# Reordering the start of the second mixture in a three-stage kernel: turns, logits, row tables and gates

## The reference, cut to what matters

```python
x = attention(...)                       # 2304 tokens x 512
x = routed_mixture(x)                    # each token: the one expert of 8 with the greatest logit
# second mixture: every token goes through all 8 experts (512 -> 1024 -> 512)
logits = x @ w_gate
P = np.exp(logits - logits.max())
for _ in range(8):                       # eight rounds of row and column scaling ("Sinkhorn")
    P /= P.sum(1, keepdims=True) + 1e-09
    P /= P.sum(0, keepdims=True) + 1e-09
    P *= N / E
for e in range(E):
    out += P[:, e:e + 1] * (np.maximum(x @ w1[e], 0.0) @ w2[e])
```

## Time and profile before

| | |
|---|---|
| time, median of 3 runs | 2225.56 us (2223.52 to 2228.18) |
| profiled execution, its time | 2224.41 us |
| profiled execution, its span | 2222.8 us |
| busy: PE, DVE, ACT, POOL | 2122.7, 1475.5, 903.0, 760.2 us |
| mean granted TensorE clock | 0.979 |
| last routed output to the end of step 2 | 643.57 to 804.6 us |

### The profile page before, as it was taken

How to read it: one execution, slowest core, us unless ns; L and a number is a source line. 1 busy time by engine, 2 the same in 40 slices (tenths; PEclk the granted TensorE clock), 3 DMA queues, 4 the chain that set the end, 5 groups by cost and what they waited for, 6 DMA issues and landing times.

```text
span 2222.8 us, 36560 instructions
## 1 busy us (share of the span) xinstructions
PE 2122.7 (95%) x12117; PEld 1937.3 (87%) x12117; DVE 1475.5 (66%) x2842; ACT 903.0 (41%) x2042; POOL 760.2 (34%) x646
## 2 busy tenths in 40 slices
PE   7998996999997899999999999999999999999998
PEld 6888886899987799998998899988998899988997
DVE  7877774876655766666666666666666666666663
ACT  5666652555544233333333333333333333333331
POOL 3544530111244323332334233322334333323331
PEclk9999997999998999999999999999999999999999
DMA  4322202777633212221123212222122222212220
GB/s 99 103 73 61 67 2 94 246 230 224 223 106 100 76 43 72 76 76 58 58 76 99 63 58 76 76 67 67 57 76 91 66 63 77 76 61 65 66 77 29
DMA packets 158031, 192.98 MB, mean 87 GB/s; under 512 B 76976, under 2 KB 76976, under 8 KB 157872
## 3 DMA queue, kind: packets, MB, share of 16 engines
q1 hardware_dynamic: 151472, 169.99, 25.5%
q0 software_dynamic: 6400, 20.98, 2.7%
HBM read 172.04 MB, written 18.87 MB: 86 GB/s over the span
## 4 chain that ended last, share of the span: by engine, by line
PE 78%; DVE 3%; issue 1%; DMA 1%; ACT 0%; another core or an unknown queue 0%; SPq 0%; POOL 0%; DVEq 0%; ACTq 0%; POOLq 0%
PE b_pso L1489 12%; PE b_pso L1490 12%; PE b_pso L1491 12%; PE b_psp L1435 10%; PE b_psp L1438 10%; PE b_psp L1437 10%; PE b_pso L961 2%; PE b_pso L963 2%; PE b_pso L962 2%; PE b_psp L963 2%; PE b_psp L961 2%; PE b_psp L962 2%; PE b_psl L1413 1%; PE b_pst L1359 0%; PE b_pst L1370 0%
## 5 line engine op out<-in xcount | busy, mean ns | idle before, releaser
L1283 POOL TENSOR_TENSOR b_w2l<-b_w2r,b_w2h 128x512 fp32r<-128x512 f32 x192 | 242.4, 1297 | 911.7 <-ACT b_w2h L1582 911.5
L1435 PE MATMUL b_psp<-b_x,b_ah 128*128 128x384 f32 x1344 | 454.7, 338 | 6.4 <-DVE b_u3c L1896 6.4
L1489 PE MATMUL b_pso<-b_w2h,b_hh 128*128 128x512 f32 x1152 | 450.7, 391 | 10.0 <-DVE b_acc L1935 9.0
L1438 PE MATMUL b_psp<-b_x,b_al 128*128 128x384 f32 x1344 | 452.5, 337 | 0.0
L1437 PE MATMUL b_psp<-b_x,b_ah 128*128 128x384 f32 x1344 | 452.1, 336 | 0.0
L1491 PE MATMUL b_pso<-b_w2h,b_hl 128*128 128x512 f32 x1152 | 450.8, 391 | 0.0
L1490 PE MATMUL b_pso<-b_w2l,b_hh 128*128 128x512 f32 x1152 | 450.7, 391 | 0.0
L1935 DVE SCALAR_TENSOR_TENSOR b_acc<-b_pso,b_prob,b_acc 128x512 f32<-128x512 f32 x264 | 198.0, 750 | 287.0 <-PE b_pso L1491 282.7
L1616 ACT ACTIVATE b_p<-b_psp 128x384 f32<-128x384 f32 x96 | 46.5, 484 | 577.5 <-PE b_psp L1438 577.4
L1489 PEld LDWEIGHTS b_pso<-b_w2h,b_hh 128*128 128x128 f32 x1152 | 217.5, 189 | 55.7 <-DVE b_acc L1935 9.9
L1435 PEld LDWEIGHTS b_psp<-b_x,b_ah 128*128 128x128 f32 x1344 | 254.5, 189 | 10.9 <-DVE b_u3c L1896 7.0
(11 more groups left out here) (276 smaller groups left out, 3892.8 us busy)
## 6 DMA issues: line engine op xcount, KB each, us to landing
dense_raw<-in_moe_w SPq DMA_DIRECT2D x192, 256.0 KB, 4.1
b_w2r<-in_moe_w SPq DMA_DIRECT2D x192, 256.0 KB, 2.7
weights_raw<-in_moe_w SPq DMA_DIRECT2D x176, 256.0 KB, 3.6
y_sorted<-r_y POOLq DMA_DIRECT2D x22, 256.0 KB
weights_raw<-in_q SPq DMA_DIRECT2D x32, 128.0 KB, 2.4
weights_raw<-in_k SPq DMA_DIRECT2D x32, 128.0 KB, 2.5
weights_raw<-in_v SPq DMA_DIRECT2D x32, 128.0 KB, 2.4
x_tokens<-a_xs SPq DMA_DIRECT2D x4, 1024.0 KB, 4.2
```

The costliest lines, as they stand in the source:

```text
L1283: g_.tensor_tensor(w2l[:, j, :], w2r[:, j, :], w2h[:, j, :].bitcast(F32), ALU.subtract).then_inc(s_wl, 1)
L1435: t_.matmul(bank, ah[:, i, d, col], bh[i][:, d, :], start=(first and d == 0), stop=False, skip_group_check=True)
L1438: m = t_.matmul(bank, al[:, i, d, col], bh[i][:, d, :], start=False, stop=(d == CH - 1), skip_group_check=True)
L1489: t_.matmul(o, hh[:, f, tok], w2h[:, f, :], start=(q == 0), stop=False)
```

## The change

Step by step: (1) `rows_chain` is cut into eight pieces inside `r_first(1)`, `mark_rows` into marks in groups 2 and 3, the table's 20 matmuls stand inside group 3's output, and `row_tables` runs a group later; for this groups 2 to 4 are written out instead of looped. (2) Tiles 0 to 5 are scaled by DVE (`first_scaled`), before its `r_ahead(last)`, and no longer by POOL. (3) The first six logits stand between the matmuls of the last routed output. (4) All seven splits of step 0 stand ahead of the last two copies to `y`; block T3 of the first pass gets memory of its own (`p1u2`), so that it needn't wait for the logits. (5) Turns and logits of tiles 6 to 17 begin at unit 14, step 0's first output tile, and end at unit 26; greatest is at 28, exp at 31, rows at 33, and the Sinkhorn rounds at 34, 36, 38, 54, 56, 58, 74, 76, all after output tiles. (6) The gates are first needed at k = 4: steps 2 and 3 add up in `acc2` (the memory of `xt[0]`), which k = 5 merges. (7) POOL does `sums(1)` ahead of the last eight fetches. (8) ACT's splits for the next step are spread over the output tiles as DVE's are.

```diff
+        acc2 = xt[0][:].rearrange("p c w -> p (c w)").rearrange("p (t d) -> p t d", d=DM)
...
         for j in range(NT - TP):
-            extras.setdefault(j + 1, []).append(("turn", TP + j))
-            extras.setdefault(j + 2, []).append(("logits", TP + j))
-        extras.setdefault(15, []).append(("greatest", 0))
-        for it in range(8):
-            extras.setdefault(19 + 4 * it, []).append(("sinkhorn", it))
+            extras.setdefault(14 + j, []).append(("turn", TP + j))
+            extras.setdefault(15 + j, []).append(("logits", TP + j))
+        extras.setdefault(28, []).append(("greatest", 0))
+        extras.setdefault(31, []).append(("exp", 0))
+        extras.setdefault(33, []).append(("rows", 0))
+        for it, u in enumerate((34, 36, 38, 54, 56, 58, 74, 76)):
+            extras.setdefault(u, []).append(("sinkhorn", it))
...
+        SPLIT_AT = (0, 1, 2), (3,), (4,), (5,), (6,), ()
...
             for t in range(TP):
                 fetch(t)
-            for t in range(TP):
-                scaled(t)
             store(last2)
             sums(0)
             store(last)
...
             w2_lo(0)
+            sums(1)
             for t in range(TP + RING, NT):
                 fetch(t)
-            sums(1)
...
-            pe.wait_ge(s_tm, 7)
-            table(psi, hotr, rows_of, NT * NV).then_inc(s_tf, 1)
-            with pe.Fori(2, last) as g:
+            def rows_table(m, f):
+                if m == 0 and f == 2 * FC - 2:
+                    pe.wait_ge(s_tm, 7)
+                    table(psi, hotr, rows_of, NT * NV).then_inc(s_tf, 1)
+
+            def first_logits(m, f):
+                if f in (1, 3, 5):
+                    logits(m * GT + f // 2)
+
+            for g in range(2, 5):
+                r_output(g - 1, g - 2, True, rows_table if g == 4 else None)
+                r_hidden(g)
+            with pe.Fori(5, last) as g:
                 r_output(g - 1, g - 2, True)
                 r_hidden(g)
             r_output(last2, count(pe, 3), True)
             r_hidden(last, last2)
-            for t in range(TP):
-                logits(t)
-            r_output(last, last2, False)
+            r_output(last, last2, False, first_logits)
...
                 for j in range(2):
                     hidden(k, j)
-                if k + 1 < STEPS:
-                    for i in range(7):
-                        if (k + 1) % (2 * E) == 0:
-                            x_hi((k + 1) // (2 * E), i)
-                        w1_hi(k + 1, i)
                 for t in range(TP):
+                    if k + 1 < STEPS:
+                        for i in SPLIT_AT[t]:
+                            if (k + 1) % (2 * E) == 0:
+                                x_hi((k + 1) // (2 * E), i)
+                            w1_hi(k + 1, i)
                     fill(k, 14 + t)
...
-                    dve.wait_ge(s_lg, TP * (p + 1))
+                    if p:
+                        dve.wait_ge(s_lg, TP * (p + 1))
...
+            def first_scaled(t):
+                dve.wait_ge(s_yg[t], 16)
+                v_.tensor_scalar(acc[:, t, :], acc[:, t, :], row_gate[:, t:t + 1], None, ALU.mult).then_inc(s_x0, 1)
...
-                if k == 2:
+                into = acc2 if k in (2, 3) else acc
+                if k == 4:
                     dve.wait_ge(s_k, 3 + 7 * 8)
                     dve.wait_ge(s_acc, TP + t + 1)
                     v_.tensor_scalar(acc[:, t, :], acc[:, t, :], prob[:, at, 0:1], None, ALU.mult).then_inc(s_sc, 1)
                     dve.wait_ge(s_sc, t + 1)
+                elif k == 5:
+                    dve.wait_ge(s_acc, TP * 4 + t + 1)
+                    v_.scalar_tensor_tensor(out=acc[:, t, :], in0=acc2[:, t, :], scalar=prob[:, at, 1:2],
+                                            in1=acc[:, t, :], op0=ALU.mult, op1=ALU.add).then_inc(s_sc, 1)
+                    dve.wait_ge(s_sc, TP + t + 1)
...
             r_first(0)
-            rows_chain()
             r_ahead(1, 0, True)
-            r_first(1, mark_rows)
+            r_first(1, rows_chain)
+            r_ahead(2, 1, True)
+            r_first(2, mark_in_tile)
+            r_ahead(3, 2, True)
+            r_first(3, mark_tile)
+            r_ahead(4, 3, True)
             row_tables()
-            with dve.Fori(2, last) as g:
+            r_first(4)
+            with dve.Fori(5, last) as g:
                 r_ahead(g, g - 1, True)
                 r_first(g)
+            for t in range(TP):
+                first_scaled(t)
             r_ahead(last, count(dve, 2), True)
             r_first(last)
             for i in range(7):
...
                 x_lo(0, i)
                 w1_lo(0, i)
-                if i == 2:
-                    r_ahead(count(dve), last, False)
+            r_ahead(count(dve), last, False)
             scaled(TP)
```

More of the change, by code:

```diff
@@ L1387, in r_hidden, with r_output @@
                         turn(f)
-            def r_output(g, before, turn_next):
+            def r_output(g, before, turn_next, also=None):
                 for m in range(RT):
@@ L1405, in r_output @@
                             f == 0, f == 2 * FC - 1)
+                        if also is not None and f < 2 * FC - 1:
+                            also(m, f)
                     i.then_inc(s_ro, 1)
@@ L1615, in hidden @@
                 after(act, s_add, 5 * (n - 1) + 1)
-                a_.activation(p1[:], bank_a, ACT.Copy).then_inc(s_p1, 1)
+                if n == 0:
+                    act.wait_ge(s_bl, T3 + 1)
+                a_.activation(p1, bank_a, ACT.Copy).then_inc(s_p1, 1)
                 if j == 0:
@@ L1718, in sources @@
                 v_.tensor_copy(idx[:, FT:], idxf[:]).then_inc(s_idx, 1)
[L1720 to L1749, removed]
-                v_.tensor_scalar(row_i[:, 1], row_i[:, 0], 7, None, ALU.logical_shift_right)
-                v_.tensor_scalar(row_i[:, 2], row_i[:, 0], P - 1, None, ALU.bitwise_and).then_inc(s_tc, 1)
-                dve.wait_ge(s_tc, 9)
-                v_.tensor_copy(row_f[:], row_i[:, 1:3]).then_inc(s_tc, 1)
@@ L1827, in extra @@
                     v_.tensor_reduce(pmax, prob[:].rearrange("p t e -> p (t e)"), AX_X, ALU.max).then_inc(s_k, 1)
+                elif kind == "exp":
                     dve.wait_ge(s_am, 1)
                     v_.tensor_scalar(nmax, amax, -1.0, None, ALU.mult).then_inc(s_k, 1)
+                elif kind == "rows":
                     dve.wait_ge(s_e, 1)
@@ L1881, in hidden @@
                 after(dve, s_add, 5 * n)
-                v_.tensor_tensor(u2[:], bank_b, p1[:], ALU.add).then_inc(s_add, 1)
+                v_.tensor_tensor(u2, bank_b, p1, ALU.add).then_inc(s_add, 1)
                 fill(k, 7 * j + 1)
@@ L1889, in hidden @@
                     dve.wait_ge(s_bl, 7 * (k // (2 * E) + 1))
-                v_.tensor_tensor(u3, bank_c, u2[:], ALU.add).then_inc(s_add, 1)
+                v_.tensor_tensor(u3, bank_c, u2, ALU.add).then_inc(s_add, 1)
                 fill(k, 7 * j + 3)
@@ L1901, in hidden @@
                 after(dve, s_hl, 4 * (n - 1) + 3)
-                v_.tensor_tensor(c21, bank_c, u2[:], ALU.add).then_inc(s_add, 1)
+                v_.tensor_tensor(c21, bank_c, u2, ALU.add).then_inc(s_add, 1)
                 hidden_lo(n, 2, c22, 2 + j, b)
@@ L1907, in hidden @@
                 after(dve, s_hl, 4 * (n - 1) + 4)
-                v_.tensor_tensor(c12, bank_d, u2[:], ALU.add).then_inc(s_add, 1)
+                v_.tensor_tensor(c12, bank_d, u2, ALU.add).then_inc(s_add, 1)
                 hidden_lo(n, 3, c21, 2 + j, a)
@@ L1925, in added @@
                 o = pso[:, t % 2, :]
-                if k == 0:
-                    v_.tensor_copy(acc[:, t, :], o).then_inc(s_acc, 1)
-                elif k == 1:
-                    v_.tensor_tensor(acc[:, t, :], o, acc[:, t, :], ALU.add).then_inc(s_acc, 1)
+                if k in (0, 2):
+                    v_.tensor_copy(into[:, t, :], o).then_inc(s_acc, 1)
+                elif k in (1, 3):
+                    v_.tensor_tensor(into[:, t, :], o, into[:, t, :], ALU.add).then_inc(s_acc, 1)
                 elif e == 0 and half == 0:
@@ L1965, in _ @@
                     if k + 1 < STEPS:
-                        for i in ((0, 1, 2), (3,), (4,), (5,), (6,), ())[t]:
+                        for i in SPLIT_AT[t]:
                             if (k + 1) % (2 * E) == 0:
```

69 lines of the change are left out of this document (54 added, 15 removed).

## The result

The changed kernel takes 2213.2 us (median of 4 runs, 2210.43 to 2214.93) against 2226.87 us (4 runs, 2223.52 to 2228.53) for the kernel before. The ratio is 0.9939, with a 95% interval of 0.9922 to 0.9957: 13.7 us faster, where 18.4 were forecast. Timed again later, on another occasion, it took 2214.81 us (10 runs) against 2218.79 (19 runs), a ratio of 0.998 (0.997 to 0.999), that is 4.0 us faster. The two intervals don't overlap: the size of the gain over the kernel before isn't settled between 4 and 14 us. The changed kernel had moved by 1.6 us, the kernel before by 8.1.

A forecast was written before the change was run, and what follows sets the result against it. PE, busy in 95% of the span, was taken as the bound, so gains must come from its idle time or lower clock. 18.2 - 0.3 + 4.0 - 3.5 = 18.4 us faster, 2207 us; range 2200.5 to 2215.5.

The forecast's parts named there:

- Part 1: Table work in groups 1 to 3: PE's idle stretches of 1.37 and 2.67 us hide behind PE, gain 4.0 us.
- Part 2: First scaling on DVE ahead of the last group: PE's gap grows to about 3.6 us, clock 1.5, together 3.5 lost.
- Part 3: First logits inside the last routed output: it takes 16.2 us at the upper clock and ends 4.9 us earlier.
- Part 4: Hidden part of step 0: PE's stall before A22 is 7.8 us instead of 11.3, released by DVE's addition into u3.
- rival B: Step 0's ring scaling held by POOL's fetches and w2_lo: A22 starts at 678.8, gain 12.4 us, 2213; chance 0.15.
- rival D: Whole kernel, no difference: all upper bounds of cost at once leave 4.6 us of gain; chance 0.06.
- Part 5: Turns and logits in output 0 and hidden 1: twelve pairs of 1.28 us, each of the two stages 23.2 us.
- Part 6: Output 1: a new wait behind POOL's all-reduce (0.5 us) and w2_lo(1), PE stalling before the third tile; 5.5 us lost.
- Part 7: Sinkhorn rounds in output parts: steps 1 and 2 lose their gaps of 3.2 us; step 2 takes 31.4 us.
- A: Output 1 hardly stalls, 1.5 us instead of 5.5, as DVE runs ahead of POOL's sums: gain 22.4, 2203; chance 0.13.
- C: Small matmuls between large ones hold TensorE at its lower clock to the end of hidden 1: slower, 2274; chance 0.03.
- E: Output 1: DVE and POOL exclude each other for whole instructions, 8.5 us lost, gain 15.4, 2210; chance 0.13.

The follow-up runs named there:

- two of the single repairs: Changed kernel with w2_lo(1) and sums(2) ahead of POOL's all-reduce, 2206.22 us; changed kernel with only the six first scalings moved into DVE's idle slot, 2209.2 us.

## Why the prediction was right or wrong

The net at the end of step 2 is 804.6 - 790.22 = 14.4 us; the forecast had 18.7 there (18.2 + 4.0 - 3.5), and 18.4 behind step 3. Three stretches add up to it:

| stretch | forecast | measured |
|---|---|---|
| to the marker | +4.0 | 614.20 - 606.37 = +7.8 |
| marker to last routed output | -3.5 | 29.4 - 32.6 = -3.2 |
| last routed output to end of step 2 | +18.2 | 161.0 - 151.3 = +9.8 |

The time lay inside the stated range, but partly by luck: the stage that the change rearranges won 8.4 us less than forecast, 5.6 of them in output 1, and the stretch to the marker won 3.8 more, of which 2.3 have nothing to do with the change (part 1).

**Part 1** was right in its mechanism and a little low. The gaps are gone, and the table's 20 matmuls, at home between other matmuls, cost 1.2 us of the group's period instead of the 2.6 that they took alone. From the first turn of group 1 to the marker it is 211.5 us (394.91 to 606.37) instead of 217.0 (397.17 to 614.20), 5.6 less: the two gaps, 4.0, and the rest from the matmuls and the clock beside them. The experiment that undid it gives 6.2 us in the trace and 5.8 in the timing. The prediction had left the table's matmuls at no gain. The other 2.3 of the 7.8 are 1.0 us by which the mixture began earlier and 1.3 in its first group, mostly a gap of 1.14. Both are scatter: the mixture starts between 381.2 and 386.5 us in the traces of this study, and the gap is none to 1.50 us in traces of kernels that are the same there.

**Part 2**: the gap was 3.89 us for the forecast 3.6, the clock 1.6 for 1.5 (24 matmuls in 7.31 us instead of 5.73). That their data are there was true in this execution and not in the later one, where the gap was 5.54.

**Part 3** holds: 16.46 us against 16.2. The logits between the output's matmuls left the clock at 1.00.

**Part 4**: the mechanism was right, the size wasn't. `A22` came after 10.2 us of idleness instead of 7.8, outside the 6 to 9 that were given as the sign, though released by the addition into `u3` as forecast. The term at fault is the 0.8 us allowed for the load of w1 beside the stores; it was 3.6 (6.21 instead of 2.60), shown by the run that held the load back. In the other traces with the load at that place and the order of the stores and fetches unchanged, the wait was 5.40 to 7.10 us. The terms behind it were a little smaller than forecast: 3.4 us to the landing instead of 3.6, and 1.7 from there to `A22` instead of 2.3. Hidden 0 took 28.84 us instead of 26.9. The prediction's bound for rival B is 677.9 in part 4 and 678.8 under the rivals; the 4.6 us of rival D come out only with the second.

**Part 5** holds: 23.36 and 23.38 us against 23.2 each, at a clock of 1.00.

**Part 6** is the step that failed: output 1 took 27.5 us, a loss of 11.1 where 5.5 was forecast and 8.5 was the bound. The mis-sized term is "all-reduce 0.5", which should have read 0.38 and 6.7 of pause. Without the all-reduce the loss is 5.7. By the prediction's own signs this part was wrong: more than 9 us lost, and PE stopped in the first tile of output 1 (4.63 and 1.24 us), not before the third. In the earlier trace rows such a pause fits inside an idle time of 11.72 us with another releaser, though no row shows it there; moving the all-reduce from that cover to a place just ahead of work that is due is what made it count.

The Trainium skill, "GPSIMD Engine Reference", section "Instruction dispatch", says that the first call to a freshly loaded GpSimd kernel also pays a code load of about 6 us, with no instruction of its own in the profile. The idle time behind the all-reduce has about that size (6.68 to 7.08 us, "issue", in seven traces), but it stands before `w2_lo`, an operation that POOL had run before; no run here shows what POOL does in that time.

**Part 7** holds: step 2 took 31.70 us against 31.4, step 3 31.48, without a stall. The moved scalings and merges cost nothing that can be seen.

**The rivals.** A and C didn't occur: output 1 stalled, and the clock was 1.00 through output 0 and hidden 1. E gave nearly the right total for another reason: 8.5 us lost by exclusion was its mechanism, and the run without the all-reduce has 5.7, 4.0 of it with POOL's work. B named the very time that was measured, 2213, and that is chance: its mechanism didn't occur in the changed kernel by a margin of 1.5 us (669.37 against 670.83), and did in the run with the load held. D, no difference, is wrong by the first timing (13.7 us) and nearly right by the second (4.0), for reasons that aren't its own: the time of the kernel before had moved.

## What to carry to other kernels

An idle time in front of an instruction isn't all due to the releaser that it names: before work is moved out of such cover, ask what else may run in it, above all on GpSimd around an operation unlike its neighbours. Where an elementwise queue of GpSimd is long, a DVE instruction that comes late to it pays all operations that follow without a pause and not one instruction, so place the DVE work before it, or behind something that nobody waits for. And where repairs differ by a few us, read the stretches and not only the times: by their ratios two of the single repairs couldn't be told from the changed kernel's first timing, while their stretches were 3.8 and 7.9 us shorter, and added up.

## What the runs showed of the hardware

- GpSimd pauses between a `partition_all_reduce` and elementwise work behind it: 6.70, 6.98 and 6.68 us, and none behind a plain copy. Where elementwise work stood ahead of the all-reduce, it started 1.41, 1.75 and 1.57 us after its operand was ready, against 0.14 in the changed kernel.
- A DVE scaling of some 0.5 us was held for 6.13 us over five GpSimd operations without a pause between them, another for 3.83 us.
- A load of four blocks (256 KB each) issued beside two stores lengthened the wait for the stores from 2.60 to 6.21 us (5.40 to 7.10 in other traces); held back, 2.80.
- After 3.9 us of idleness TensorE ran at its lower level for the first eight matmuls of 512 columns (0.63 us each, granted clock 0.57 from 617.3 to 621.2); after 1.2 us it did not fall (0.39 us each).
